# Attention and two MoE layers in one kernel: order of the loads, filler matmuls, and narrower masks and first scores

## The reference, cut to what matters

```python
batch, n_heads, seq, head_dim = (2, 8, 768, 64)
n_global, n_local = (8, 96)
scores = scale * np.matmul(q, k.transpose(0, 1, 3, 2))          # scale = 1/8
rel = pos[:, None] - pos[None, :]
is_global = pos[None, :] < int(n_global)
is_local = (rel >= 0) & (rel < int(n_local))
keep = is_global | is_local
dist = np.where(is_global & ~is_local, float(n_local), np.abs(rel))
scores = np.where(keep, scores - slopes[:, None, None] * dist, -1e9)
a = softmax(scores)                                             # sum + 1e-9
x = (a @ v)                       # as 1536 tokens x 512
h = x @ w_in1;  x = (h * sigmoid(h)) @ w_out1                   # 512 -> 2048 -> 512
h = x @ w_in2;  y = (h * clip(h + 3, 0, 6) / 6) @ w_out2
```

## Time and profile before

| | us |
|---|---|
| runs | 596.42, 596.89, 597.41 |
| profiled execution | 596.89 |
| its span, first to last instruction | 595.1 |
| TensorE busy | 586.8 (99%) |
| VectorE, ScalarE, GpSimd busy | 365.7, 336.1, 267.5 |
| granted TensorE clock, mean | 1.000 |

### The profile page before, as it was taken

The page is one execution under the profiler, slowest core; times in us unless marked ns, Lnnn a source line. Parts: engine busy times, 40 slices in busy tenths (PEclk is TensorE's granted clock), DMA queues, the critical chain, the costliest instruction groups (busy, mean ns, idle before and its releaser), DMA issues.

```text
span 595.1 us, 9691 instructions
## 1 busy us (share of the span) xinstructions
PE 586.8 (99%) x3477; PEld 523.7 (88%) x3477; DVE 365.7 (61%) x680; ACT 336.1 (56%) x661; POOL 267.5 (45%) x279
## 2 busy tenths in 40 slices
PE   8999899999999999999999999999999999999998
PEld 5777688999999999999999999888888988899996
DVE  6777677768555768557544685475558665554331
ACT  5988785544444756555544675444547655555441
POOL 4665776559433334377333244394332343331110
DMA  8435331222222122122222132112221262111002
GB/s 352 152 128 203 121 121 39 106 72 62 81 72 72 36 70 72 72 70 73 72 71 72 36 105 72 60 48 72 70 72 35 72 204 74 48 65 37 1 0 106
DMA packets 14595, 50.05 MB, mean 84 GB/s; under 512 B 1618, under 2 KB 1874, under 8 KB 14546
## 3 DMA queue, kind: packets, MB, share of 16 engines
q1 hardware_dynamic: 14258, 48.63, 23.8%
q10 hardware_dynamic: 288, 0.79, 0.4%
HBM read 46.27 MB, written 3.15 MB: 83 GB/s over the span
## 4 chain that ended last, share of the span: by engine, by line
PE 92%; DMA 4%; DVE 2%; issue 1%; SPq 0%; ACT 0%; POOL 0%; DVEq 0%
PE ps L1043 39%; PE ps L1130 23%; PE ps L1121 14%; PE ps L1122 7%; PE ps L981 3%; DMA q_raw<-in_qT 3%; PE ps L1015 3%; PE ps L991 3%; DVE g_lo L696 1%; DMA k_raw<-in_kT 1%; PE ps L1000 1%; DVE g_f L553 1%; DVE wi_lo L526 0%; ACT g_hi L901 0%; DVE negs L565 0%
## 5 line engine op out<-in xcount | busy, mean ns | idle before, releaser
L382 POOL TENSOR_TENSOR wo_lo<-wo_raw,wo_hi 128x1024 fp32r<-128x1024 f32 x32 | 77.0, 2407 | 261.1 <-ACT wo_hi L830 255.9
L1043 PE MATMUL ps<-x_hi,wi_hi 128*128 128x384 f32 x448 | 151.2, 337 | 0.7 <-DVE c_sb L543 0.3
L1043 PE MATMUL ps<-x_hi,wi_lo 128*128 128x384 f32 x448 | 150.0, 335 | 0.0
L1043 PE MATMUL ps<-x_lo,wi_hi 128*128 128x384 f32 x448 | 150.0, 335 | 0.0
L543 DVE TENSOR_TENSOR c_sb<-ps,p_c 128x384 f32<-128x384 f32 x64 | 35.6, 557 | 159.6 <-PE ps L1043 159.4
L810 ACT ACTIVATE p_c<-ps 128x384 f32<-128x384 f32 x64 | 31.5, 492 | 128.9 <-PE ps L1043 128.5
L1043 PEld LDWEIGHTS ps<-x_hi,wi_hi 128*128 128x128 f32 x448 | 84.1, 188 | 4.8 <-issue 1.2
L1043 PEld LDWEIGHTS ps<-x_hi,wi_lo 128*128 128x128 f32 x448 | 84.1, 188 | 0.7
L1043 PEld LDWEIGHTS ps<-x_lo,wi_hi 128*128 128x128 f32 x448 | 84.1, 188 | 0.0
L1130 PE MATMUL ps<-wo_hi,g_lo 128*128 128x512 f32 (+1 forms) x194 | 76.3, 393 | 0.0
L1130 PE MATMUL ps<-wo_lo,g_hi 128*128 128x512 f32 (+1 forms) x194 | 76.3, 393 | 0.0
(11 more groups left out here) (104 smaller groups left out, 1082.9 us busy)
## 6 DMA issues: line engine op xcount, KB each, us to landing
wi_raw<-in_w_in SPq DMA_DIRECT2D x32, 512.0 KB, 3.4
wo_raw<-in_w_out SPq DMA_DIRECT2D x32, 512.0 KB, 3.4
v_raw<-in_v SPq DMA_DIRECT2D x8, 704.0 KB, 4.2
k_raw<-in_kT SPq DMA_DIRECT2D x8, 464.0 KB, 4.9
out_y<-y_out SPq DMA_DIRECT2D x11, 256.0 KB, 4.1
q_raw<-in_qT SPq DMA_DIRECT2D x6, 384.0 KB, 5.4
q_raw<-in_qT ACTq DMA_DIRECT2D x2, 384.0 KB, 4.1
out_y<-y_out SPq DMA_DIRECT2D x2, 128.0 KB, 1.9
```

The costliest lines, as they stand in the source:

```text
L382: nc.gpsimd.tensor_tensor(wo_lo[:, s % 2, :], wo_raw[:, s % 2, :], wo_hi[:, s % 2, :], ALU.subtract).then_inc(wo_lo_ok, 1)
L1043: mm = nc.tensor.matmul(p_bank(bank), w[:, s % 2, at], x[:, b, k, :], start=fresh and k == 0 and i == 0, stop=k == 1 and i == 2, skip_grou ...
```

## The change

- SP: q and k of pair `it` are issued as soon as their own wait (`s_done`) is met; v of pair `it - 1` comes behind them, with the wait that it had before. v of pair 7 comes last.
- TensorE waits for a DVE memset of 128 x 128 ones (in `y_out`) instead of POOL's identity, and its filler is five and four fp32 matmuls of ones instead of eight and five transposes.
- `glb` is computed on the two stretches of 32 columns where global keys can be; `m_base` is the sum of `rel8` and `far` everywhere, and the maximum with `glb` is taken on those stretches alone. `base_ok` counts to 2.
- The reciprocals of round 0 are taken in DVE's round 1 instead of round 2; those of round 1 stay in round 3.
- The score matmuls of a pair's first tile stream 128 columns instead of 256.

```diff
             def banded():
                 load_v(sp, 1)
                 first_w()
                 for it in range(2, NPAIR):
                     sp.wait_ge(s_done, HALF * (it - 1))
                     load_qk(sp, it)
-                    sp.wait_ge(pv_done, HALF * (it - 1))
-                    load_v(sp, it)
+                    if it > 2:
+                        sp.wait_ge(pv_done, HALF * (it - 2))
+                        load_v(sp, it - 1)
+                sp.wait_ge(pv_done, HALF * (NPAIR - 2))
+                load_v(sp, NPAIR - 1)
...
             def banded():
-                pool.wait_ge(base_ok, 1)
+                pool.wait_ge(base_ok, 2)
...
+            nc.vector.memset(y_out[:, 0, 0:P], 1.0).then_inc(idle_ok, 1)
             for h in range(2 * NH):
...
             def base():
                 rel, key, rel8, far, glb = [m[:, :] for m in m_tmp]
+                GLOB_COLS = (slice(P - GLOB, P), slice(256, 256 + GLOB))
                 dve.wait_ge(iota_ok, MW_IOTAS)
                 nc.vector.tensor_scalar(far, rel, nl, NEVER, ALU.is_ge, ALU.mult).then_inc(chain, 1)
-                nc.vector.tensor_scalar(glb, key, ng, NEVER, ALU.is_ge, ALU.mult).then_inc(chain, 1)
-                links[0] += 2
+                for at in GLOB_COLS:
+                    nc.vector.tensor_scalar(glb[:, at], key[:, at], ng, NEVER, ALU.is_ge, ALU.mult).then_inc(chain, 1)
+                links[0] += 3
                 dve.wait_ge(chain, links[0])
-                link(nc.vector.tensor_tensor(far, rel8, far, ALU.add))
-                nc.vector.scalar_tensor_tensor(m_base[:, :], glb, nums[:, 3:4], far, ALU.add, ALU.max).then_inc(base_ok, 1)
-                dve.wait_ge(base_ok, 1)
+                link(nc.vector.tensor_tensor(m_base[:, :], rel8, far, ALU.add))
+                for at in GLOB_COLS:
+                    nc.vector.scalar_tensor_tensor(m_base[:, at], glb[:, at], nums[:, 3:4], m_base[:, at], ALU.add,
+                                                   ALU.max).then_inc(base_ok, 1)
+                dve.wait_ge(base_ok, 2)
...
-                    if r >= 2:
-                        inverse(r - 2)
+                    if r == 1 or r >= 3:
+                        inverse(max(r - 2, 0))
...
             def banded():
-                act.wait_ge(base_ok, 1)
+                act.wait_ge(base_ok, 2)
...
         def _(pe):
-            pe.wait_ge(ident_ok, 2)
+            pe.wait_ge(idle_ok, 1)
             def busy(n):
                 for _ in range(n):
-                    nc.tensor.transpose(ps[:, 0, 0:P], ident[:, :], ident[:, :])
-            busy(8)
+                    nc.tensor.matmul(ps[:, 0, 0:P], y_out[:, 0, 0:P], y_out[:, 0, 0:P], start=True, stop=True)
+            busy(5)
             pe.wait_ge(ones_ok, 1)
             pe.wait_ge(row_ok, 2)
             nc.tensor.matmul(ps[:, 1, 0:4], ones[:, :], cnt[:, 4:8], start=True, stop=True).then_inc(rows_ok, 1)
-            busy(5)
+            busy(4)
+            pe.wait_ge(ident_ok, 2)
...
-                    first = KS * (t - 1) + GLOB if t else 0
+                    first, width = (KS * (t - 1) + GLOB, 256) if t else (0, P)
                     for h in range(2):
-                        mm = nc.tensor.matmul(s_bank(u, h), q_raw[it % 2][D * h:D * h + D, P * t:P * t + P],
-                                              k_raw[it % 2][D * h:D * h + D, first:first + 256], start=True, stop=True)
+                        mm = nc.tensor.matmul(s_bank(u, h)[:, 0:width], q_raw[it % 2][D * h:D * h + D, P * t:P * t + P],
+                                              k_raw[it % 2][D * h:D * h + D, first:first + width], start=True, stop=True)
```

More of the change, by code:

```diff
@@ L159, in x_quad @@
             return x_raw[:, KT * b + 2 * (quad // 2):KT * b + 2 * (quad // 2) + 2, TB * (quad % 2):TB * (quad % 2) + TB]
-        words_in = sem("words_in"); ones_ok = sem("ones_ok"); row_ok = sem("row_ok"); rows_ok = sem("rows_ok"); ident_ok = sem("ident_ok"); iota_ok = sem("iota_ok")
+        words_in = sem("words_in"); ones_ok = sem("ones_ok"); row_ok = sem("row_ok"); rows_ok = sem("rows_ok"); ident_ok = sem("ident_ok"); idle_ok = sem("idle_ok"); iota_ok = sem("iota_ok")
         chain = sem("chain"); flag_ok = sem("flag_ok")
```

## The result

The changed kernel takes 592.13 us in the median (591.84 to 592.52, 4 runs) against 596.65 for the kernel before in the same comparison; the ratio is 0.9924 with a 95% interval of 0.9907 to 0.9942. The forecast was 591.7 us, in a range of 590.3 to 593.7. The profiled execution took 592.52 us, its span is 590.8. So the gain is 4.4 us between the two profiled executions and 4.5 between the medians, where 5.15 were forecast.

What follows compares the result with a forecast made beforehand. PE (TensorE), busy in 99% of the span, was taken as the bound. Loads 2.4, narrow scores 1.25 and opening 1.5 sum to 5.15 us off 596.89, giving 591.7 us, range 590.3 to 593.7.

Steps and rivals of the forecast that it cites:

- Loads: SP's queue in the attention rounds: q and k issued ahead of v end five PE waits, worth 2.4 us.
- Scores of first tiles: PE in six rounds: 128 instead of 256 columns save 0.21 us a round, 1.25 us in all.
- Opening: Start of the kernel up to the first values on PE: fillers, masks and early inverse bring them 1.5 us sooner.
- fillers and the level: PE's opening: scores start near 5.75, the clock level rises inside scores(0), DVE's first reduction comes 0.45 us earlier.
- the all-low sum: Opening with everything at the low clock level: DVE's first reduction moves from 7.75 to 7.57, 0.2 us earlier.
- ACT's gap behind round 1: ACT's 0.65 us idle in the opening, released by DVE's negmax, goes because scores(1) and scores(2) run at the high level.
- Early inverse: Opening: round 0's reciprocals taken in r = 1 let POOL's spread come up to 1.55 us sooner; ACT's 0.44 us idle goes.
- Masks: DVE in the opening: shorter mask instructions are worth nothing, or up to 0.4 us if the level rises very early.
- The handover to the next stage: After the rounds: x_lo ends 0.9 us before PE's product that reads it; the whole lead is passed on.
- rival 3: Lead not passed on: q and k still late, 594.1 us, or the next stage holds it back, 593.4; 10%.
- the second: Rival on the opening: the clock level rises no earlier than before, opening gains 0.6 us, time 592.6 us; 13%.
- The rule on transposes: PE's fillers: true matmuls of ones instead of transposes should bring the level's rise forward, perhaps ahead of the scores.

Runs made afterwards that it cites:

- loads_only: The kernel before with only SP's new order of loads: 593.76 us, ratio 0.9954.
- opening_only: The changed kernel with the old order of loads and 256 columns in all scores, leaving fillers, masks and early inverse: 595.91 us, ratio 0.9991.
- loads_and_narrow: The kernel before with the new order of loads and the narrow first-tile scores, its opening parts unchanged: 592.00 us, ratio 0.9915.
- after_again: The changed kernel run once more, unaltered: 592.24 us, ratio 0.9923.
- after_long_fill: The changed kernel with 5 and 13 filler matmuls of ones instead of 5 and 4: 593.46 us, ratio 0.9945.

## Why the prediction was right, and where a term was off

- **Loads: right.** Forecast 2.4 of at most 2.5; the stretch of loads_only is 2.43 us shorter. The v loads kept their time and nothing came in the waits' place; ACT did have the room (busy 49.99 of 56.70 us).
- **Scores of first tiles: right.** 0.21 us a round was forecast, 0.20 measured; with the waits the rounds lost 3.69 us of the forecast 3.65.
- **Opening: mis-sized, 0.69 instead of 1.5 us.** The step that failed is the one on fillers and the level: "I take it inside scores(0)". In the changed kernel's two traces, and in three of its variants with the same first fillers and `busy(4)` or `busy(3)`, the level rose at 8.0 or later, when scores(0) was over, and so it didn't help the first reduction. Only in opening_only, whose scores(0) streams all columns and lasts longer, did it rise inside scores(0), at 7.5; there the first reduction came at 8.06, 0.26 sooner than the 2.25 us from the start of the scores to it in the earlier trace rows would give. The fillers were also priced too low. Their spacing of 0.213 us holds, but the first record of each of the two groups takes some 0.37 us before the next where a transpose took 0.27, and the first score starts 0.35 us behind the last filler record, more than one spacing. The scores start at 6.07, not 5.75, and the first reduction is at 7.90, where the all-low sum gave 7.57. These two, 0.33 for the fillers and 0.27 for the level, are 0.6 of the 0.8 missing. The rest is ACT's gap behind round 1, of which 0.39 of 0.65 us stayed, as round 1's scores also ran at the low level.
- **How the 0.69 divides.** About half of it isn't the work of the three opening parts: loads_and_narrow, which leaves them out and has its level at 10.4 as before, has its first values at 17.33, 0.35 sooner than before. It has narrow scores in scores(0), and its scores started 0.16 us sooner (5.34).
- **Early inverse: right in its mechanism.** ACT's gap of 0.44 went; alone it is worth 0.56 us in the first values, by one pair of traces.
- **Masks: right**, nothing.
- **The handover to the next stage** passed everything on: x_lo ends at 87.38 + 0.96 = 88.34 us and its product starts at 89.26, so the 0.9 us of the earlier trace rows are still there. The chain moved with PE, which is why rival 3 failed. DVE's row:

```profile
87.38 0.96 DVE L548 TENSOR_TENSOR x_lo<-x_t,x_hi 128x768 fp32r<-128x768 f32 x1 [1.06 <-ACT x_hi L815]
```

- **The rivals.** What came in the profiled execution was the second in all but name: the level rose 0.4 us sooner than before, but behind scores(0) and scores(1), where it could help neither; opening 0.6 and 592.6 forecast, 0.69 and 592.52 measured. It had been given 13%. The median of 592.13 lies inside the forecast's own range of 591.2 to 592.3 all the same. The profiled execution itself lies just outside that range; the median falls inside it with three executions of which there is no trace. So that this number fell inside, with the opening's term 0.8 too high, is in part luck; that it came near is owed to the loads and the narrow scores. With after_again's level at 8.0 the opening's lead was 1.15, still below 1.5.
- **The rule on transposes**, that they don't count as activity of TensorE in the way matmuls do ("TensorE: Matmul & The Clock Gate" in the Trainium skill, Part 4: PE-mode transpose), does not fit this case. In loads_only the level was high before the first score, when only transposes and one small matmul had run. The same page (Part 1) also says that the point of the rise differs between runs of one kernel. That fits: 10.0 and 8.0 us with identical programs, and 10.4 and 5.0 with the same instructions ahead of the scores.

## What to carry to other kernels

When a queue issues loads with waits between them, look for a load whose own wait is met and that stands behind another's; moving it ahead cost nothing here and brought more than half of the gain. In a stage whose bound is one engine, columns that nobody reads were worth their full time (0.20 us of 0.21 a round); an instruction shortened on an engine that then waits was worth nothing. Don't judge a change to the first microseconds from one trace: compare the same program's executions first. A filler that ends after the data has landed delays the first real work (by 0.43 us for the last matmul of ones), though no time here shows the loss.

## What the runs showed of the hardware

- The point at which TensorE's level rises differs between executions of the same program. The changed kernel had it at 10.0 and 8.0 us, the one without fillers at 12.0 and 10.8. Over all kernels, fillers of transposes had it at 10.4, 5.0, 9.7, 10.4 and 9.1 us, fillers of ones at 10.0, 7.5, 8.0, 9.1, 8.1, 7.2 and 9.8. What sets the point stays open. The two executions without fillers ran on different chips, but on one chip it was at 5.0 and 9.7 with the same instructions ahead of the scores. Whether ones are better than transposes stays open: the ranges overlap, and five and seven traces don't settle it.
- In the changed kernel a rise 2.0 us sooner (8.0 against 10.0) brought the first values 0.46 us sooner (16.53 against 16.99). That is ACT's gap of 0.39 us and little more: in after_again ACT has no gap from 8.23 on, so its own work set the rest. A rise ahead of all scores (5.0 against 10.4, with the opening of before) brought 1.37.
- The granted clock stood as 1.00 in every stretch in which records were spaced as at 1.2 GHz, so that number doesn't show the level; the same form of instruction at two times does.
- A true fp32 matmul of 128 columns took two records, 0.43 us at the low level and 0.22 at the high (spacing in after_long_fill 0.21 and 0.11 a record); a transpose took one.
